# Order of roundings and low parts in a fused attention, gating and expert-attention kernel; zeros of a mask table on another engine

## The reference

```
scores = scale * (q @ k.transpose(0, 2, 1))
scores = np.where(causal, -1000000000.0, scores)
a = np.exp(scores - scores.max(-1)) ; a /= a.sum(-1) + 1e-09
out += mask[..., None] * w[:, :, kk:kk + 1] * (a @ v @ wo[e])
```

## Time and profile before

| | |
|---|---|
| runs | 496.26, 496.90, 498.81 us, median 496.9 |
| profiled execution | 496.05 us, its span (first to last instruction) 494.2 us |
| busy | PE 96%, DVE 65%, ACT 55%, POOL 43% of the span |
| granted TensorE clock | 1.000 over the whole span |
| chain that ended last | PE 73%, DVE 14%, ACT 7%, issue 3%, POOL 2% |

### The profile page before, as it was taken

The page is one execution under the profiler, slowest core; times in us unless marked ns, Lnnn a source line. Parts: engine busy times, 40 slices in busy tenths (PEclk is TensorE's granted clock), DMA queues, the critical chain, the costliest instruction groups (busy, mean ns, idle before and its releaser), DMA issues.

```text
span 494.2 us, 10632 instructions
## 1 busy us (share of the span) xinstructions
PE 474.0 (96%) x3794; PEld 404.1 (82%) x3794; DVE 320.9 (65%) x1247; ACT 271.7 (55%) x822; POOL 213.6 (43%) x378
## 2 busy tenths in 40 slices
PE   8689989999999999999999999999999999999996
PEld 5457989899776789999776779999876779999874
DVE  6886875257778855437778865436777975335783
ACT  5667563246676744235666654335666663335663
POOL 4494628222344526742253525760443442461431
PEclk9999999999999999999999999999999999999999
DMA  7927520003201073002311063001311000000111
GB/s 235 320 55 217 201 86 0 1 2 76 91 22 44 2 197 91 1 1 48 109 34 44 1 184 106 0 2 40 95 44 56 1 1 2 0 2 8 42 43 54
DMA packets 33512, 31.64 MB, mean 64 GB/s; under 512 B 6002, under 2 KB 24434, under 8 KB 33460
## 3 DMA queue, kind: packets, MB, share of 16 engines
q1 hardware_dynamic: 33460, 30.97, 20.6%
HBM read 23.88 MB, written 4.72 MB: 58 GB/s over the span
## 4 chain that ended last, share of the span: by engine, by line
PE 73%; DVE 14%; ACT 7%; issue 3%; POOL 2%; DVEq 0%; POOLq 0%
PE bank L1385 16%; PE bank L1387 15%; PE bank L1386 15%; PE bank L1372 6%; PE bank L1450 6%; ACT p L825 4%; PE bank L1412 3%; DVE ring L936 3%; PE bank L1614 3%; PE bank L1629 2%; PE bank L1651 2%; DVE p L1170 2%; PE bank L1391 2%; PE bank L1392 1%; POOL ring L542 1%
## 5 line engine op out<-in xcount | busy, mean ns | idle before, releaser
L542 POOL TENSOR_SCALAR ring<-ring,r 128x128 f32<-128x128 f32 x144 | 62.4, 447 | 80.1 <-DVE r L956 79.8
L628 POOL TENSOR_SCALAR p<-p,r,wgt 128x128 f32<-128x128 f32 (+3 forms) x64 | 38.6, 616 | 92.9 <-DVE wgt_last L1217 49.9
L656 ACT ACTIVATE ring<-ring,neg 128x128 f32<-128x128 f32 x144 | 56.7, 396 | 23.9 <-DVE ring L947 19.4
L825 ACT ACTIVATE p<-p,neg 128x128 f32<-128x128 f32 (+4 forms) x72 | 41.7, 580 | 31.9 <-DVE neg L1170 31.9
L936 DVE CUSTOM_DVE_ANT_0 ring<-bank,bias 128x256 f32<-128x256 f32 (+1 forms) x128 | 43.7, 385 | 6.1 <-PE bank L1372 5.6
L1372 PE MATMUL bank<-k,q 64*128 64x256 f32 (+2 forms) x320 | 39.0, 372 | 2.8 <-DVE neg L936 2.8
L592 POOL TENSOR_TENSOR g_lo<-uT,g_hi 128x288 fp32r<-128x288 f32 x32 | 26.8, 862 | 32.1 <-ACT g_hi L791 32.1
L1385 PE MATMUL bank<-g_hi,w_c_hi 128*128 128x288 f32 x128 | 38.3, 299 | 2.1 <-DVE k_lo L1273 2.1
L1385 PE MATMUL bank<-w_spatial_hi,vn_hi 128*128 128x288 f32 x128 | 37.9, 296 | 2.3 <-DVE uT L1149 2.3
L1385 PE MATMUL bank<-x_hi,w_in_hi 128*128 128x288 f32 x128 | 38.2, 298 | 0.0
L1387 PE MATMUL bank<-x_hi,w_in_lo 128*128 128x288 f32 x128 | 37.7, 294 | 0.0
(11 more groups left out here) (193 smaller groups left out, 1447.7 us busy)
## 6 DMA issues: line engine op xcount, KB each, us to landing
v_in<-v SPq DMA_DIRECT2D x16, 256.0 KB, 3.9
out<-o_sb SPq DMA_DIRECT2D x16, 256.0 KB, 2.0
q<-qT SPq DMA_DIRECT2D x15, 256.0 KB, 4.5
k<-kT SPq DMA_DIRECT2D x15, 256.0 KB, 4.8
v_minus_v_of_tile_above<-v SPq DMA_DIRECT2D x9, 256.0 KB, 3.9
w_in_raw<-w_in SPq DMA_DIRECT2D x4, 512.0 KB, 5.7
w_cat_raw<-wcat SPq DMA_DIRECT2D x1, 1544.0 KB, 7.1
w_spatial_raw<-wsT SPq DMA_DIRECT2D x1, 1152.0 KB, 8.6
```

Of the source, the lines that this page charges most:

```text
L542: last = nc.gpsimd.tensor_scalar(p, p, r1[:, i % 2, h:h + 1], 0.0, ALU.mult, ALU.add)
L628: nc.gpsimd.tensor_scalar(p, p, r3[:, i % 2, e:e + 1], by, ALU.mult, ALU.mult).then_inc(s3_sd, 1)
L656: nc.scalar.activation(x, x, ACT.Exp, bias=neg1[:, u % SLOTS1:u % SLOTS1 + 1], scale=-1.0, accum_out=sum1[:, i % 2, h:h + 1]).then_inc(s1_ ...
L825: nc.scalar.activation(p, p, ACT.Exp, bias=neg3[:, w % 4:w % 4 + 1], scale=-1.0, accum_out=sum3[:, i % 2, es[0]:es[0] + 1]).then_inc(s3_ex, 1)
```

## The change

Four edits:

- ACT writes the zeros of the mask table before its first exponential (a broadcast copy of zeros); POOL's memset is gone and POOL waits for ACT's semaphore instead.
- The eight w_cat subtractions on DVE move from ahead of the gating loop into its steps 4 to 7, two in each, ahead of the w_outT subtraction that is there already.
- In stage 3 of each batch ACT runs high_qk(4) ahead of exp3(0) and exp3(1) instead of after them.
- ACT runs high_z(0) between exp3(8) and exp3(9) in step m = 0 instead of at the head of step m = 1. DVE's and TensorE's lists of stage 3 are as they were.

```diff
-                    link(nc.gpsimd.memset(masks[:], 0.0))
+                    pool.wait_ge(s_mz, 1)
...
+            nc.scalar.copy(masks[:].rearrange("p (a c) -> p a c", c=LAST),
+                           pt_hi[:, 0, 0:LAST].bitcast(F32).unsqueeze(1).to_broadcast([P, 1024 // LAST + 1, LAST])).then_inc(s_mz, 1)
             exp1(0, 0)
...
                 exp_logits(0)
+                high_qk(4)
                 exp3(0)
                 exp3(1)
-                high_qk(4)
                 exp3(2)
...
-                    for i in range(NT - 2):
+                    for i in range(1, NT - 2):
                         if m == DEND3[i] + 1:
                             high_z(i)
...
                     for w in units3(m):
+                        if w == 2 * E + 1:
+                            high_z(0)
                         exp3(w)
...
-                if first:
-                    for d in range(KT):
-                        dve.wait_ge(s_fsh, d + 1)
-                        nc.vector.tensor_tensor(wcat_lo[:, d, 0:CUT], wcat_raw[:, d, 0:CUT], wcat_qk_hi[:, d, :].bitcast(F32),
-                                                ALU.subtract).then_inc(s_fsl, 1)
-                    for d in range(KT):
-                        dve.wait_ge(s_fsh, KT + d + 1)
-                        nc.vector.tensor_tensor(wcat_lo[:, d, CUT:CW], wcat_raw[:, d, CUT:CW], wcat_v_hi[:, d, :].bitcast(F32),
-                                                ALU.subtract).then_inc(s_fsl, 1)
+                def low_w_cat(d, c0, c1, high, n):
+                    dve.wait_ge(s_fsh, n)
+                    nc.vector.tensor_tensor(wcat_lo[:, d, c0:c1], wcat_raw[:, d, c0:c1], high[:, d, :].bitcast(F32), ALU.subtract
+                                            ).then_inc(s_fsl, 1)
+
                 for i in range(8):
                     a, dt = divmod(i, 4)
                     c = slice(HALF * a, HALF * a + HALF)
                     if first and i >= 4:
                         d = i - 4
+                        low_w_cat(d, 0, CUT, wcat_qk_hi, d + 1)
+                        low_w_cat(d, CUT, CW, wcat_v_hi, KT + d + 1)
                         dve.wait_ge(s_fsh, 2 * KT + d + 1)
```

More of the change, by code:

```diff
@@ L274, in build @@
         s1_h2 = sem("s1_pt_second_copied")
+        s_mz = sem("causal_masks_zero")
         s_diag, s_vd, s1_cb = sem("diagonal_mask_ready"), sem("v_steps"), sem("s1_blocks_joined")
```

## The result

The changed kernel took 497.76 us (median of 20 runs, 497.3 to 499.45), the kernel before, in the same rounds, 496.85 us (20 runs, 495.23 to 498.81): a ratio of 1.0024, 95% interval 1.0013 to 1.0035. The change of 0.24% is clear of noise (the interval leaves out 1) and lies within what the prediction calls no change, but the forecast was 494.4 us in a range of 492.5 to 497.0, and the time lies above it. The profiled execution took 498.14 us against 496.05, its span 496.2 us against 494.2: 2.0 us more.

The account below looks back on a forecast made before the run. TensorE, busy 474.0 of 494.2 us, was taken as the bound, so only its gaps could be won. Terms -1.05 - 0.6 - 0.5 = -2.15 us gave 494.4 us, range 492.5 to 497.0.

Parts of the forecast that it names:

- A: Mask table zeros moved from POOL to ScalarE: TensorE's 1.44 us gap at 33.57 shrinks, -1.05 us.
- D: First batch, w_cat subtractions moved among the gatings: fold starts at 81.45 instead of 82.06, -0.6 us.
- That a group of three goes through in one piece is my choice: DVE's fold subtractions between gatings: POOL is not let in inside a group of three.
- 0.4 + 3 x 0.25 = 1.15 us of waiting: DVE's waits for POOL at the fold subtractions: 0.4 us for the first group, 0.25 for each later one.
- The undisturbed sum: DVE's fold subtractions and gatings without POOL's disturbance: last low part written at 80.3 us.
- first rival: POOL gets the port after every DVE subtraction, 73 to 84 us: change +0.55 us, 497.05 us; chance 0.14.
- The working of the bound: Upper bound at the fold: 5.2 us of POOL work, some 1.3 beside gatings, fold at 84.2, +2.1 us.
- B: high_qk(4) ahead of exp3(0) and exp3(1): gap before the seventh q/k product grows 0.53 to 0.86, +0.33 us a batch.
- C: high_z(0) between exp3(8) and exp3(9): gap before the first output product goes, -0.31 us a batch, -0.40 in the first.
- The second rival: Fold subtractions run undisturbed because POOL's casts come later: change -3.25 us, 493.25 us; chance 0.16.
- the third: Something else ends the gap at 33.57 at the same time: change -1.1 us, 495.4 us; chance 0.08.
- the last: B costs more than C returns: +0.33 us four times, change -0.35 us, 496.15 us; chance 0.12.

Follow-up runs that it names:

- Experiment 2: Changed kernel, POOL's first low part of g (first batch) held until DVE's twelve fold subtractions are done ("POOL held"): 491.87 us, ratio 0.9904.
- D alone: Kernel before with only the w_cat subtractions moved among the gating steps: 499.65 us, ratio 1.0064.
- experiment 4: Changed kernel, POOL writing zeros with a one-input instruction instead of the low parts of g in the first batch: 494.34 us, ratio 0.9940.
- experiment 1: Kernel before with one edit each: mask zeros 495.93 us, high_qk(4) early 498.23, high_z(0) early 494.46, w_cat subtractions moved 499.65.
- experiment 7: Changed kernel with low_qk(4) ahead of reciprocal3(0) and the four wide w_cat subtractions on POOL ahead of its low parts of g: 493.31 us, ratio 0.9935.

## Why the prediction was wrong

**A.** Right: -1.05 us forecast, -1.03 and -1.06 in the traces. The copy takes 1.10 us on ScalarE, in idle time ahead of the first exponential, which still starts at 5.67 (2.97 us of idle time are 1.85 now):

```profile
2.72 1.10 ACT L663 CAST causal_masks<-pt_hi 128x1088 bf16<-128x1088 f32 x1
...
5.67 0.40 ACT L657 ACTIVATE ring<-ring,neg 128x128 f32<-128x128 f32 x1 [1.85 <-DVE neg L941]
```

**D: the step that failed** is "That a group of three goes through in one piece is my choice", and the term that hangs on it, 0.4 + 3 x 0.25 = 1.15 us of waiting, which measured 3.9. The undisturbed sum was right (80.3, which is 79.5 with A's shift and the start-up; with POOL held it was 79.0, in an execution 0.52 us further ahead at that place), and DVE was late next, as put. But POOL is let in after any subtraction behind which it has an instruction ready, seven times and not four, and where it is let in DVE loses 0.61 us (once 0.25), not 0.25 to 0.4. D was forecast at -0.6 us; it came to +2.18 us at the fold's start and +1.70 by the clock. The prediction had this as its first rival, with the fold at 84.2; with A's gain and the start-up taken out, the changed kernel has 83.41 + 1.03 - 0.20 = 84.24. The working of the bound (5.2 us of POOL's work less 1.3 beside gatings, 3.9) met the measured 3.9, in part by luck: it let POOL in after each subtraction of all four groups, where the groups of the trace had 3, 2, 1 and 1 meetings. Experiment 2 shows the cause, since only POOL's time was changed.

What misled was the one pair of w_in subtractions, 1.27 us beside a POOL scaling that took 1.40. That pair is 1.27 us long in the changed kernel too, so the row was no accident; but the same two operations that would meet again had met at w_outT: of the four subtractions there two took 0.90 and 1.30 us, and these two 0.68 and 0.82, which the prediction's "0.90 or 1.30" leaves out:

```profile
78.90 0.68 DVE L1146 TENSOR_TENSOR w_outT_lo<-w_outT_raw,w_outT_hi 128x512 fp32r<-128x512 f32 x1
...
80.76 0.82 DVE L1146 TENSOR_TENSOR w_outT_lo<-w_outT_raw,w_outT_hi 128x512 fp32r<-128x512 f32 x1
```

The prediction treated them as heads of a group, since each stood alone ahead of a gating: they couldn't tell the two cases apart, and one row of another kind was let decide. By the rule of the Trainium skill ("SBUF — State Buffer", section "SBUF: two separate sides"), one instruction holds the port and the other engine waits it out, which as the prediction said gives the upper bound; the trace agrees at the twelve fold subtractions, with 0.61 us for six of the seven meetings. Why POOL wasn't let in between the two of w_in stays open.

**The clock was in no case of the prediction.** It had a gap of 1.9 us ahead of the fold and priced it as idle time alone. A gap of 2.28 us among the spatial products left the clock at 1.00, and this was taken as settled without being said. The fold's stretch lost 1.70 us behind 4.53 us of standstill in the changed kernel (1.57 of them the clock's), 2.36 behind 4.28 with D alone, and 1.68 behind 2.01 us in experiment 4. So even the first rival, with everything else right, came out 1.7 us too low. The rival's +0.55, the clock's +1.7 and B and C 0.5 better than put make +1.75, near the +2.05 of the spans. The range was drawn too narrow by the prediction's own figures as well: it is said to take in the means of all four rivals, but the first's, 497.05, lies above its end at 497.0.

**B.** Right to the step: ScalarE's order turned, DVE's didn't, the gap went from 0.53 to 0.85 us (0.86 forecast); alone it costs 1.27 us (1.32 forecast). **C.** Right in kind, too small: 0.31 was read from the bracket as all there was to win, and 0.59 came. That is the term of the sum that was mis-sized: B and C together gave -1.0 us, not -0.5. The second rival (undisturbed subtractions) describes experiment 2, not this kernel; the third (something else ends A's gap) and the last (B costs more than C returns) fell with experiment 1.

## What to carry to other kernels

When DVE's two-input operations are moved beside a run of POOL's, count one full POOL instruction after each of DVE's for as long as POOL has one ready (here seven behind twelve subtractions), not one short wait per group, and ask for whom POOL's are urgent: here nobody needed them, and one wait was worth 5.9 us by time, 5.5 in the traces. A standstill that moves to another place of the same engine can bring a fall of the clock with it there, though it brought none before: price the slow products behind it beside the idle time. When an early result is to pay, the engine that uses it has to be reordered too, and part of the gap comes back at the next waits of the same circle: here 0.50 of 0.68 us.

## What the runs showed of the hardware

- The meeting of DVE and POOL is paid by the length of the other's instruction: 0.61 us for POOL's two-input 128x288, 0.23 us for its one-input 128x288 (whose row begins while DVE's is still running, and so has a wait in it too). Their rows are 0.80 and 0.43 us where no such subtraction of DVE is beside them. DVE's 64x576 with one input, 0.46 us alone, took 1.43 us beside POOL's 1.57 us subtractions.
- TensorE's clock was at half for about 3.4 us behind the standstill of 4.53 us, and for as long behind one of 2.01 us, where it fell only 1.2 us after the fold had begun, and behind one of 3.02 us (experiment 7). Behind 4.28 us (D alone) it was at half for 6.8 us, 4.9 of them in the fold. So the length of the standstill didn't set the price. It did not fall behind 2.28 us in the kernel before, nor behind 0.63 us with POOL held. What the engine did before those gaps differed; which of it decides was not tried.
- An idle time that the trace puts ahead of a product showed less here than its removal was worth: 0.31 us shown and 0.59 gained (C), 2.28 shown and 2.51 gained among the spatial products, 0.53 shown and 0.68 gained at the seventh q/k product.
